# Nine small softmax tiles move behind the large ones in SBUF (attention and two feed-forward layers, one core)

## The reference

```
kv_pool = mean of kv over 4x4 windows             # 768 keys
k = v = kv_pool @ w_sr
a = softmax(q @ k.T / sqrt(128));  x = a @ v       # 12288 x 128
h = x @ w_in1;  g = h where h >= 1, 0 where h <= -1, else (h + 1)^2 / 4;  y1 = g @ w_out1
h = y1 @ w_in2; g = h * sigmoid(1.702 h);          y2 = g @ w_out2
```

## Time and profile before

| | |
|---|---|
| median of three runs | 1352.31 us |
| the profiled execution's own time | 1349.45 us |
| its span, first to last instruction | 1347.6 us |
| TensorE busy | 1286.5 us, 95% |
| DVE, ACT, POOL busy | 80%, 76%, 75% |
| mean granted TensorE clock | 0.985 of full speed |
| share of PE in the chain that ended last | 89% |

### The profile page before, as it was taken

How to read it: one execution, slowest core, us unless ns; L and a number is a source line. 1 busy time by engine, 2 the same in 40 slices (tenths; PEclk the granted TensorE clock), 3 DMA queues, 4 the chain that set the end, 5 groups by cost and what they waited for, 6 DMA issues and landing times.

```text
span 1347.6 us, 17170 instructions
## 1 busy us (share of the span) xinstructions
PE 1286.5 (95%) x5496; PEld 1037.6 (77%) x5496; DVE 1074.4 (80%) x1227; ACT 1021.8 (76%) x1085; POOL 1016.7 (75%) x417
## 2 busy tenths in 40 slices
PE   5486999999999999999999999999999999999988
PEld 3354888888888888888888888888888888878866
DVE  7988888897887888888888878878888888766433
ACT  3565887888778788788878787787887788796756
POOL 2755697797797797877977977977878779779760
PEclk9798999999999999999999999999999999999999
DMA  9100010010000000000000000000000000000000
GB/s 337 40 16 16 9 32 17 16 31 16 16 16 20 27 16 16 31 16 16 31 16 16 31 16 16 16 19 28 16 16 31 16 16 24 9 16 16 0 8 17
DMA packets 18605, 36.19 MB, mean 27 GB/s; under 512 B 3344, under 2 KB 3472, under 8 KB 18320
## 3 DMA queue, kind: packets, MB, share of 16 engines
q1 hardware_dynamic: 18576, 35.83, 8.0%
HBM read 29.43 MB, written 6.39 MB: 27 GB/s over the span
## 4 chain that ended last, share of the span: by engine, by line
PE 89%; DVE 4%; issue 2%; POOL 1%; DMA 1%; ACT 1%; SPq 0%; POOLq 0%; ACTq 0%; DVEq 0%
PE ps_ring L377 17%; PE ps_ring L379 17%; PE ps_ring L378 17%; PE ps_y L377 13%; PE ps_y L379 13%; PE ps_y L378 13%; DMA kv_sb<-in_kv_t 1%; DVE s_sb L765 1%; POOL g_lo L341 1%; DVE part_sum L771 1%; DVE g L822 1%; DVE g_hi L815 1%; DVE pt_lo L702 0%; SPq L249 0%; POOL w_lo L325 0%
## 5 line engine op out<-in xcount | busy, mean ns | idle before, releaser
L341 POOL TENSOR_TENSOR g_lo<-g,g_hi 128x1024 fp32r<-128x1024 f32 x192 | 524.3, 2731 | 111.3 <-DVE g L822 91.5
L334 POOL TENSOR_TENSOR g_lo<-g,g_hi 128x1024 fp32r<-128x1024 f32 x181 | 437.5, 2417 | 149.0 <-ACT g_hi L624 149.0
L815 DVE SCALAR_TENSOR_TENSOR g_hi<-g,ps_ring 128x1024 fp32r<-128x1024 f32 x192 | 234.0, 1219 | 134.8 <-ACT g L638 133.1
L622 ACT ACTIVATE g<-ps_ring 128x1024 f32<-128x1024 f32 x192 | 197.2, 1027 | 185.5 <-PE ps_ring L379 185.3
L377 PE MATMUL ps_y<-g_hi,w_hi 128*128 128x512 f32 x768 | 306.3, 399 | 9.3 <-POOL g_lo L341 7.6
L379 PE MATMUL ps_y<-g_hi,w_lo 128*128 128x512 f32 x768 | 303.4, 395 | 0.0
L378 PE MATMUL ps_y<-g_lo,w_hi 128*128 128x512 f32 x768 | 300.2, 391 | 0.0
L822 DVE SCALAR_TENSOR_TENSOR g<-g,ps_ring 128x1024 f32<-128x1024 f32 x192 | 233.0, 1213 | 0.0
L631 ACT ACTIVATE g<-ps_ring 128x1024 f32<-128x1024 f32 x192 | 197.8, 1030 | 19.1 <-POOL g_lo L341 12.3
L638 ACT ACTIVATE g<-g 128x1024 f32<-128x1024 f32 x192 | 203.8, 1061 | 5.4
L624 ACT ACTIVATE g_hi<-ps_ring 128x1024 fp32r<-128x1024 f32 x192 | 195.7, 1019 | 5.4 <-PE ps_y L379 5.4
(11 more groups left out here) (85 smaller groups left out, 1743.2 us busy)
## 6 DMA issues: line engine op xcount, KB each, us to landing
kv_sb<-in_kv_t SPq DMA_DIRECT2D x12, 512.0 KB, 8.6
q_sb<-in_q_t SPq DMA_DIRECT2D x24, 256.0 KB, 3.6
key_max<-max_row SPq DMA_DIRECT2D x24, 256.0 KB, 3.4
inv_sum<-inv_row SPq DMA_DIRECT2D x24, 256.0 KB, 3.1
out_t<-y_sb SPq DMA_DIRECT2D x24, 256.0 KB, 3.4
w_raw<-in_moe_w_in SPq DMA_DIRECT2D x2, 1024.0 KB, 8.4
max_row<-max_turned SPq DMA_DIRECT2D x24, 2.0 KB, 1.3
inv_row<-inv_turned SPq DMA_DIRECT2D x24, 2.0 KB, 1.3
```

The lines of the kernel that those rows point to most:

```text
L334: nc.gpsimd.tensor_tensor(g2_lo[:, slot, :], g2[:, slot, :], g2_hi[:, slot, :].bitcast(F32), ALU.subtract).then_inc(g2_lo_done, 1)
L341: nc.gpsimd.tensor_tensor(g1_lo[:, slot, :], g1[:, slot, :], g1_hi[:, slot, :].bitcast(F32), ALU.subtract).then_inc(g1_lo_done, 1)
L622: nc.scalar.activation(g2[:, slot, :], ps_h2(k), ACT.Gelu_apprx_sigmoid).then_inc(g2_done, 1)
L815: nc.vector.scalar_tensor_tensor(out=g1_hi[:, uu % 2, :], in0=g1[:, uu % 2, :], scalar=1.0, in1=ps_h1(k), op0=ALU.min, op1=ALU.max).then_i ...
```

## The change

Nine declarations move from between q_lo and inv_sum to the end of the list. Nothing else is edited: the instructions, their order on every engine, their shapes and their waits stay as they were; only the addresses in them differ.

```diff
         q_lo = sb(ctx, "q_lo", [C, T], F32R)
-        part_max = sb(ctx, "part_max", [P, KC, QB])
-        fold_max = sb(ctx, "fold_max", [P, QUADS, QB])
-        row_max = sb(ctx, "row_max", [SQ, SQ])
-        max_turned = sb(ctx, "max_turned", [SQ, SQ])
         key_max = sb(ctx, "key_max", [P, T])
-        part_sum = sb(ctx, "part_sum", [P, KC, QB])
-        fold_sum = sb(ctx, "fold_sum", [P, QUADS, QB])
-        row_sum = sb(ctx, "row_sum", [SQ, SQ])
-        inv_turned = sb(ctx, "inv_turned", [SQ, SQ])
-        eps = sb(ctx, "eps", [SQ, QB])
         inv_sum = sb(ctx, "inv_sum", [P, T])
...
         y2_sb = sb(ctx, "y2_sb", [C, T])
+        part_max = sb(ctx, "part_max", [P, KC, QB])
...
+        eps = sb(ctx, "eps", [SQ, QB])
```

More of the change, by code:

```diff
@@ L113, in encoder_kernel @@
         y2_sb = sb(ctx, "y2_sb", [C, T])
+        part_max = sb(ctx, "part_max", [P, KC, QB])
+        fold_max = sb(ctx, "fold_max", [P, QUADS, QB])
+        row_max = sb(ctx, "row_max", [SQ, SQ])
+        max_turned = sb(ctx, "max_turned", [SQ, SQ])
+        part_sum = sb(ctx, "part_sum", [P, KC, QB])
+        fold_sum = sb(ctx, "fold_sum", [P, QUADS, QB])
+        row_sum = sb(ctx, "row_sum", [SQ, SQ])
+        inv_turned = sb(ctx, "inv_turned", [SQ, SQ])
+        eps = sb(ctx, "eps", [SQ, QB])
         with ExitStack() as banks:
```

## The result

The changed kernel takes 1338.03 us (median of four runs, 1335.35 to 1338.39), the kernel before beside it 1352.45. The ratio is 0.9894, with a 95% interval of 0.9875 to 0.9913: about 1.1% faster. The profiled execution took 1335.35 us (before 1349.45).

The account below looks back on a forecast made before the run. TensorE was taken as the bound, with matmuls back to back. Savings of 17.5 us less 1 us of waits gave 16.5: from 1349.45 to 1333.0, with the median's 2.9 us offset 1335.8 us; range 1331 to 1344.5.

Parts of the forecast that it names:

- TensorE's distance from start to start is the time: Steady stretch, 150 to 1190 us: nobody makes TensorE wait, so time is 4524 matmuls at 229.9 ns each.
- All streamed slices at one remainder bring all matmuls to 226.7 ns: Matmuls at full clock: with x and y1 at remainder 128 too, all reach the score/value block's rate, saving 17.5 us.
- Rival 1: Layer matmuls: only x and y1 get faster, g stays slow; 8.2 us saved, 1344.1 us; chance 0.10.
- 1 us of new waits: TensorE behind POOL's g2_lo: margin 0.42 us shrinks to 0.10, so few waits, 1 us in all.
- under some us: Sign in the profile after: PE's waits for POOL's L334 or L341 stay under some us in total.
- The sum by places: Savings by stretch: 14.4 us from 150 to 1190, 0.1 to 1200, 1.6 to 1290, 0.8 after, 0.6 before 150; sum 17.5.
- own upper end of 1339: Top of the forecast's own range, 1331 to 1339 us, meant to allow 3 us of new waits.
- rival 2: POOL's run with thin margin: one more meeting with DVE per tile gives about 1353 us, fewer meetings 1344; chance 0.06.
- rival 3: TensorE's operand reads: addresses change nothing, by the rule or because higher digits count; 1352.3 us; chance 0.06.
- rival 4: Layer matmuls: x and y1 at new places break the step each time, 234.0 ns each, 1365.8 us; chance 0.06.
- The median 2.9 us above the profiled execution: Whole kernel: offset between the shown runs' median and the profiled execution, added to 1333.0 to give 1335.8 us.

Follow-up runs that it names:

- the shifts tried: Changed kernel with an unused tile of 32, 64, 128, 256 or 512 bytes ahead of x_sb: spans 1351.5, 1347.6, 1344.9, 1335.2 and 1333.4 us.
- The early q_lo: Changed kernel with POOL making q_lo ahead of g1_lo in step 3, not behind it: 1358.36 us, ratio 1.0052 without the two longest executions.
- the weights alone: Changed kernel with unused tiles of 64 bytes ahead of w_hi and behind w_lo, so only the layers' weights lie off the common place: span 1339.7 us.

## Why the prediction was right

It gave 1335.8 us, a range of 1331.0 to 1344.5, and 0.87 for faster. Measured: 1338.03 us. By its steps:

- *TensorE's distance from start to start is the time; the other engines are not late.* Right: same busy time of DVE, ACT and POOL, 14.6 us less of PE.
- *All streamed slices at one remainder bring all matmuls to 226.7 ns.* Right: 5.44 us for 24, as forecast; x_hi 389/389/389. Rival 1 (g keeps its slowness) fell in the same rows. The reading behind it was right in part: I had the remainder among streamed operands, with weights at rest; it is the distance to the stationary one (A1), and of the shifts tried the multiples of 256 bytes are free, not only those of 2048. For this change both readings forecast the same, since it brings all of them to 128.
- *1 us of new waits.* This was the term most mis-sized: 28 places of some 0.11 us, 3.1 to 3.3 us. I took the margin, 0.42 us, to the matmul; what waits for POOL is its weight load, whose margin was 0.20 us. A TensorE that is 0.32 us earlier must then wait, and it does in each tile. I also looked at one place of a tile only; the g2_lo that TensorE takes up in step 2 makes it wait in every second tile. The sign that waits stay "under some us" did not come true for the weight loads (7.1 us of idle time), only for what TensorE lost by them.
- *The sum by places.* The stretch from 150 to 1190 us gained 49 matmuls, 11.1 us, which is 14.4 less the 3.3 of the waits. The ramp gained nothing: x_hi's first matmul of the stretch starts at 153.7 and not at 153.5, where I had 0.6 saved. Behind 1190 us there are 3.2 us, where I had 0.1 + 1.6 + 0.8 = 2.5, but 1.6 of them are the clock's dip. So the addresses give 12.5 us against 16.5 forecast. That 17.5 less the waits comes so near to the 14.1 measured is in part luck.
- *The range.* Its own upper end of 1339 doesn't follow: 17.5 - 3 = 14.5 us from 1352.3 gives 1337.8, and 1338.03 was measured. The wide range holds it in any case, by rival 1's 1344.5.
- *POOL takes the gain back* (rival 2): in small, by margin, not by one more meeting with DVE. L341's mean is 2728 ns (before 2731). The early q_lo showed that the danger was there: seven stalls of DVE made the kernel slower than before the change.
- *The places don't matter* (rival 3), with the rule that the prediction quotes from the Trainium skill ("SBUF — State Buffer", section "Who interferes with whom") that TensorE's two read ports are independent: it would have given 0. The runs do not agree: unused tiles alone move the span from 1333.4 to 1351.5 us.
- *The new places never let the reads settle* (rival 4) fell with 5.44 us for a full step; that would have taken over 5.54.
- *The median 2.9 us above the profiled execution*: 2.7 here, in another set of runs 0.3. It was an offset of three executions, and that it came again was luck.

What stays open is the mechanism below the distance: the runs show that the relative place of the two operands decides and that 256 and 512 bytes of shift are free, not what in the chip makes it so. That the two reads fall into a step with each other was not shown.

## What to carry to other kernels

When TensorE is the bound and its matmuls stand back to back, compare the time under way of equal shapes by tile: here groups that differed by a fixed few ns, with min and max equal, differed by address. For matmuls like these (128x128 by 512 columns of 4 bytes, each with its own weight load) put streamed and stationary operands at one remainder after division by 256 bytes; small tiles go behind the large ones or are filled up. Other shapes and types were not tried. And ask of a faster TensorE which hand-over had little to spare, and take the margin to the weight load, not to the matmul. Before two spans are subtracted, compare the granted clock stretch by stretch: here it made 1.6 of 14.1 us.

## What was not expected

- The shifts differ in price: in the 1040 us of the steady stretch 32 bytes cost 67 matmuls, 64 cost 49, 128 cost 44, the weights alone against all else 23.
- A wait of TensorE as short as these shows in no idle column of PE, only as a weight load's wait and a matmul of 0.45 to 0.50 us in place of 0.39.
- A DVE instruction with two operands in SBUF took 6.46 us for 1.21 us of work beside three POOL instructions without a gap.
